# Loading the first layer's input by column planes, each with a semaphore of its own, instead of by token blocks

## The reference

```python
k_p = k.reshape(B, H, S // 8, 8, D).mean(axis=3)         # B, H, S, D = 8, 8, 576, 64
v_p = v.reshape(B, H, S // 8, 8, D).mean(axis=3)
attn = softmax(q @ k_p.T / sqrt(D))                       # 8 sequences, 8 heads
x = (attn @ v_p) reshaped to (4608, 512)

h = x @ w_in                                              # 512 -> 2048
g = maximum(h, 0) + alpha * minimum(h, 0)
y = g @ w_out                                             # 2048 -> 512

logits = normalized(y) @ normalized(expert_emb).T / tau   # 8 experts
e = argmax(logits); gate = softmax(logits)[e]
out = gate * (maximum(y @ w1[e], 0) @ w2[e])              # 512 -> 1024 -> 512
```

## Time and profile before

| | |
|---|---|
| median of 3 runs | 1415.29 us |
| the three runs | 1414.76, 1415.29, 1419.02 us |
| the profiled execution's own time | 1414.76 us |
| its span, first to last instruction | 1413.0 us |
| PE busy | 1394.3 us, 99% of the span |
| DVE busy | 813.8 us, 58% |
| POOL busy | 702.1 us, 50% |
| ACT busy | 687.2 us, 49% |
| mean granted TensorE clock | 0.995 of full speed |
| transfers | 152.54 MB in 212679 packets |

### The profile page before, as it was taken

The page is one execution under the profiler, slowest core; times in us unless marked ns, Lnnn a source line. Parts: engine busy times, 40 slices in busy tenths (PEclk is TensorE's granted clock), DMA queues, the critical chain, the costliest instruction groups (busy, mean ns, idle before and its releaser), DMA issues. The chain is left out here.

```text
span 1413.0 us, 21354 instructions
## 1 busy us (share of the span) xinstructions
PE 1394.3 (99%) x7261; PEld 1146.8 (81%) x7261; DVE 813.8 (58%) x1498; ACT 687.2 (49%) x1016; POOL 702.1 (50%) x613
## 2 busy tenths in 40 slices
PE   8999999999999999999999999999999999999997
PEld 7887888888888888888888888888888788887886
DVE  7655788777768867777677486770002900065660
ACT  5333443443443533434434312545666666666664
POOL 5552244354352453542343332476666866678763
PEclk9999999999999999999999999899999999999999
DMA  8544143252252242423322221263433964369541
GB/s 259 164 117 150 47 110 92 55 135 73 70 124 73 68 131 68 122 65 60 75 60 46 67 75 68 90 231 83 96 91 92 247 161 97 79 144 252 141 116 27
DMA packets 212679, 152.54 MB, mean 108 GB/s; under 512 B 142812, under 2 KB 175580, under 8 KB 212448
## 3 DMA queue, kind: packets, MB, share of 16 engines
q1 hardware_dynamic: 71488, 99.20, 22.3%
q10 hardware_dynamic: 133056, 33.05, 14.0%
q0 software_dynamic: 8032, 18.93, 4.1%
HBM read 92.34 MB, written 29.43 MB: 86 GB/s over the span
## 5 line engine op out<-in xcount | busy, mean ns | idle before, releaser
L852 PE MATMUL h_ps<-x_hi_in,weight_parts 128*128 128x512 f32 x1144 | 373.6, 390 | 0.0
L1858 POOL TENSOR_TENSOR g_lo<-g_full,g_hi 128x512 fp32r<-128x512 f32 x144 | 202.3, 1405 | 335.6 <-ACT g_hi L1543 335.5
L868 PE MATMUL y_ps<-weight_parts,g_hi 128*128 128x512 f32 x1152 | 359.7, 393 | 1.7 <-POOL g_lo L1858 1.7
L868 PEld LDWEIGHTS y_ps<-weight_parts,g_hi 128*128 128x128 f32 x1152 | 213.0, 188 | 47.4 <-issue 1.9
L852 PEld LDWEIGHTS h_ps<-x_hi_in,weight_parts 128*128 128x128 f32 x1144 | 214.8, 188 | 44.4
L975 PE MATMUL y_ps<-weight_parts,x_hi_in 128*128 (+1 forms) x1032 | 244.7, 393 | 0.6 <-issue 0.4
L1543 ACT ACTIVATE g_hi<-g_full 128x512 fp32r<-128x512 f32 x144 | 90.9, 632 | 302.3 <-PE y_ps L868 210.2
L975 PEld LDWEIGHTS y_ps<-weight_parts,x_hi_in 128*128 128x128 f32 x1032 | 194.8, 189 | 42.1 <-issue 1.9
L868 PE MATMUL y_ps<-weight_parts,g_lo 128*128 128x512 f32 x576 | 224.5, 390 | 0.0
L852 PE MATMUL h_ps<-x_lo_in,weight_parts 128*128 128x512 f32 x572 | 222.6, 389 | 0.0
L1164 DVE TENSOR_SCALAR g_full<-h_ps,alpha 128x512 f32<-128x512 f32 x144 | 107.9, 749 | 193.0 <-PE h_ps L852 190.3
(11 more groups left out here) (233 smaller groups left out, 1798.7 us busy)
## 6 DMA issues: line engine op xcount, KB each, us to landing
shared<-in_w SPq DMA_DIRECT2D x8, 2048.0 KB
emb_all<-in_w SPq DMA_DIRECT2D x8, 2048.0 KB
y_dram<-y_rows SPq DMA_DIRECT2D x9, 1024.0 KB, 4.3
shared<-in_q SPq DMA_DIRECT2D x34, 256.0 KB, 2.9
shared<-in_v SPq DMA_DIRECT2D x29, 288.0 KB
x_dram<-shared SPq DMA_DIRECT2D x32, 256.0 KB, 3.2
y_rows<-x_dram SPq DMA_DIRECT2D x32, 256.0 KB, 5.0
shared<-in_k SPq DMA_DIRECT2D x26, 288.0 KB, 3.5
```

Of the source, the lines that this page charges most:

```text
L852: mm = pe.matmul(h_ps[:, f % 2, :], w[:, k, f * P:(f + 1) * P], x[:, k, :], start=(n == 0), stop=(n == 3 * DC - 1))
L868: mm = pe.matmul(y_ps[:, j, :], a[:, f % 2, j * P:(j + 1) * P], w[:, f, :], start=(f == 0 and n == 0), stop=(f == FC - 1 and n == 2))
L1858: pool.tensor_tensor(gl[:, f % 2, :], g_full[:, f % 2, :], gh[:, f % 2, :].bitcast(F32), ALU.subtract).then_inc(gl_done, 1)
```

## The change

`load_x` now waits once, for the store of the last of the four steps, and then issues four transfers of one feature chunk each: transfer k brings the [128, 512] plane of 128 features and all 512 tokens of the tile, one run of 512 floats (2048 bytes) on each partition. The bytes and the number of transfers are the same. Each plane has its own semaphore, and each `x_hi(i, k)` waits for its own plane; the first also waits, as before, for PE.

```diff
-        x_loaded = sem("x_loaded")
+        x_loaded = [sem(f"x_loaded{k}") for k in range(DC)]
...
+        xc_dram = x_dram.rearrange("(c p) s -> c p s", p=P)
...
-                for j in range(TB):
-                    sp.wait_ge(stored, 16 * (last_step(i) - TB + j + 2 - FIRST))
-                    first = i * TT + j * QB
-                    sp.dma_start(y[:, :, j * QB:(j + 1) * QB], xs_dram[:, :, first:first + QB]).then_inc(x_loaded, 16)
+                sp.wait_ge(stored, 16 * (last_step(i) + 1 - FIRST))
+                for k in range(DC):
+                    sp.dma_start(y[:, k, :], xc_dram[k, :, i * TT:(i + 1) * TT]).then_inc(x_loaded[k], 16)
...
             def x_hi(i, k):
 
+                act.wait_ge(x_loaded[k], 16 * i)
                 if k == 0:
-                    act.wait_ge(x_loaded, 16 * TB * i)
                     act.wait_ge(h_done, FC * i)
                 act.activation(xh[:, k, :], y[:, k, :], ACT.Copy).then_inc(xh_done, 1)
```

## The result

The changed kernel is slower: 1426.59 us median (1418.38 to 1434.65, 20 runs) against 1416.72 us (1410.53 to 1421.89, 20 runs), a ratio of 1.0065 with an interval of [1.0051, 1.0079]. I had forecast 1413.6 us. The profiled execution took 1430.08 us with a span of 1428.4 us; it is 3.5 us above the median of its kernel.

What follows compares the result with a forecast made beforehand. PE, busy 1394.3 of 1413.0 us, was taken as the bound, helped only where it idles. Removing the first round's gap gave 1415.29 − 1.67 = 1413.6 us, all other terms nothing; range 1411.0 to 1418.0.

Steps and rivals of the forecast that it cites:

- The gap at the end of tile 0: First round: planes land after 3.4 us, PE's wait for g_lo at chunk 15 disappears, saving 1.67 us; chance 0.67.
- my 123.3: End of tile 0: g_hi of chunk 15 was forecast to start on ACT at about 123.3 us.
- The other seven rounds: Later x loads: planes land before x_hi needs them, cover 4.5 us after a 5.7 us landing; cost nothing, bounds 0 and 0.
- none below −1.67, since nothing else waits there: End of tile 0: lower bound of the gap's term, a gain of at most 1.67 us.
- the bound above, 2.3: End of tile 0: with 7.7 us to land, the second plane is in at 127.0, costing 2.3 us.
- v on SP: Other seven rounds: SP held 1.4 us longer, hidden because the load of v is issued at 213.76 anyway; cost nothing.
- The rival of late planes: End of tile 0, x_hi: planes land later than the old fourth block, 1415.7 to 1417.6 us; chance 0.08.
- its threshold, 9.6 us for over 0.3%: End of tile 0: second plane's landing time from which the kernel is over 0.3% slower; chance 0.02 beyond it.
- Being slower by over 0.3%: Whole kernel: outcome given 0.07, summed from late planes 0.02, clock low for longer 0.04 and scatter 0.01.
- The clock at the turn to the experts: About 901 to 911 us: PE's 5.1 us clock loss vanishes (1408.5, chance 0.04) or lasts longer (1418.7 if doubled, 0.06).
- The packets: x loads: 16384 packets of 512 B replaced by 4096 of 2048 B, 200391 packets in all.
- The sign to look for: Behind 131 us: a growing difference between the kernels was named as one sign that the forecast is wrong.

Runs made afterwards that it cites:

- e2: Kernel before with planes in round 1 alone, old blocks and wait in rounds 2 to 8; ratio to before 0.9968, 1415.46 us median.
- e11: The kernel of e2 (planes in round 1 alone) measured a second time; ratio to before 0.9979, 1415.52 us.
- e4: Changed kernel with the old blocks in round 1 and planes in rounds 2 to 8; ratio to before 1.0076.
- e6: The changed kernel run again, unaltered, for a second profile and time; ratio to before 1.0041.
- e3: Changed kernel, but in rounds 2 to 7 planes stand behind v's load and wait for the first transposing transfer; ratio to before 1.0051.
- e12: Changed kernel, but in rounds 2 to 7 the first transposing transfer waits until the last plane has landed; ratio to before 1.0080.
- e8: Changed kernel with loads of v cut to 16 of 72 partitions from the third sequence on; ratio 1.0262, with another routing.

## Why the prediction was wrong

1. *The gap at the end of tile 0.* Right. The planes landed in 2.6 to 4.4 us, median 3.5, for my 3.4; the new tile starts 1.58 us earlier for my 1.67; e2 and e11 show it alone, e4 without it. One reading in it was wrong without harm: I wrote that ACT could round chunk 15 from 122.04 on, but g_hi also waits for PE's second layer of chunk 13 (l2_done), and the trace shows it released by that at 123.43. That this is my 123.3 is luck; the planes were there earlier.
2. *"The other seven rounds ... Cost nothing, bounds 0 and 0, unless a load takes 10 us."* This is the step that failed. Those rounds cost 10.9 us in the profiled execution, though no load in it took 10 us (the slowest 9.7; 10.3 in e6). I asked whether x_hi would find its planes in time, and it did: no x_hi of rounds 2 to 8 waited for a load. I took the landing of 5.7 us from the old trace, in which three of four blocks had their start before the transposing transfer, and did not ask what else was released by the store I moved them behind. The wait for `stored` in `turn_plane` was in the kernel's text, and its queue not in my list. So the landing, taken as 5.7, was up to 9.7, and the path that I followed, x_hi, was not the one that mattered: the delay reached PE through two other queues, ACT's, which waits for the transposed plane, and POOL's, which waits for v.
3. *"none below −1.67, since nothing else waits there"* was read from one execution. With the same blocks in round 1, e4 had a wait of 3.2 us and a fall of the clock behind it, so the term can be worth more; and the bound above, 2.3, looked at round 1 only, where no transposing transfer runs.
4. *v on SP.* I had priced the issue time of 1.4 us, hidden, and not the landing behind 1 MB. POOL's waits for v from 131 to 700 us rose from 14.3 to 35.6 us.
5. *The rival of late planes* had the right sign (slower) in the wrong place: it spoke of round 1. That its threshold, 9.6 us for over 0.3%, lies beside the slowest plane, 9.7, is chance; it was a price for the second plane of round 1, which took 2.9. Being slower by over 0.3% had been given 0.07 in all. *The clock at the turn to the experts* took the same in the two profiles: after the change it was 0.90, four times 0.50 and 0.54 of full in stretches of 2 us from 909 to 921 us, 5.1 us as in the earlier trace rows. But it differs by the execution: in the profile of e2 it stayed at 1.00 through the turn, and in that of e11, the same kernel, it cost 5.1 us again. So this term belongs to the scatter and not to the change. What the change added were falls behind PE's gaps, 1.7 us in round 2.
6. *The packets:* 200391, as predicted; fewer packets meant no faster loads where it counted.
7. The sign to look for was named rightly, "a difference between the kernels that grows behind 131 us".

What stays open: why a transposing transfer and loads slow each other down, how much the run length adds, and what decides in which executions the clock falls, in the rounds and at the turn to the experts; that is a part of the 16 us by which the changed kernel's executions differ.

## What to carry to other kernels

A wait that several transfers share, on an event that another queue waits for too, makes them start together: before moving a transfer behind an event, list everything else that the event releases, on all queues. Blocks sent as their data comes cost more packets but keep only the last one at the crowded place; here the planes belong in the one round where the wait ended on the engine that bounds the kernel (e2 and e11, 0.9968 and 0.9979). Separating two transfers by a wait on a busy in-order engine moves the loss (e3, e12).

## What the hardware showed unexpectedly

A transposing transfer of one plane mostly takes 3.0 to 3.1 us. With four loads of 256 KB released 0.7 us before it, it took 8.2 to 8.9 us in the profile after and the loads up to 9.7; in e4 and e6, with the same release, 6.6 to 10.6 and up to 10.7. With a start of 1.8 us for the loads (round 7 after) it took 5.4, with 1.4 to 1.7 and little v (rounds 3 to 6 of e8) 5.0 to 6.0, with 2.8 (round 2 of e8) 4.0. With a plain copy of as many bytes, copies took at most 5.7 and loads at most 6.9. In the stretch in which they shared, the transfer engines were 0.86 busy and moved 157 GB/s, at the same place before 0.85 and 216. The store in front also took 5.7 us with v and k beside it and 3.1 with little v, so the distance between the two releases is itself set by other traffic.
